# Query scalings of chunk 8 shared between two prologue chunks, and three weight splits in two parts each, in a recurrent attention and two-MoE kernel

## What is computed

```python
# q, k, v, alpha: (4, 8, 768, 48)
for t in range(S):
    state = alpha[:, :, t, :, None] * state + np.einsum('bhd,bhe->bhde', k[:, :, t], v[:, :, t])
    y[:, :, t] = np.einsum('bhd,bhde->bhe', q[:, :, t], state)
# x: (3072, 384) from y
p = domain_probs / (domain_probs.sum(-1, keepdims=True) + 1e-09)
for e in range(4):
    out += p[:, e:e + 1] * (np.maximum(x @ w1[e], 0.0) @ w2[e])
# second block, on out
h = x @ w_in
out = ((h * np.clip(h + 3.0, 0.0, 6.0) / 6.0) @ w_out)
```

## Time and profile before

| what | value |
|---|---|
| time, median of 3 runs | 1395.45 us (1394.85 to 1399.09) |
| time of the profiled execution | 1396.57 us |
| its span | 1394.7 us |
| PE busy | 1371.8 us, 98% of the span |
| POOL busy | 790.4 us, 57% |
| DVE busy | 698.2 us, 50% |
| ACT busy | 534.9 us, 38% |
| mean granted TensorE clock | 0.995 of full |

### The profile page before, as it was taken

How to read it: one execution, slowest core, us unless ns; L and a number is a source line. 1 busy time by engine, 2 the same in 40 slices (tenths; PEclk the granted TensorE clock), 3 DMA queues, 4 the chain that set the end, 5 groups by cost and what they waited for, 6 DMA issues and landing times.

```text
span 1394.7 us, 31927 instructions
## 1 busy us (share of the span) xinstructions
PE 1371.8 (98%) x12476; PEld 1116.7 (80%) x12476; DVE 698.2 (50%) x1401; ACT 534.9 (38%) x992; POOL 790.4 (57%) x860
## 2 busy tenths in 40 slices
PE   7799999999999999999999999999999999999998
PEld 5578888888888888888888888888888888888887
DVE  8766665445454545454544445454445333333333
ACT  2233333333354333354433335533335433335543
POOL 7866666555655565556555655565555444444442
PEclk9899999999999999999999999999999999999999
DMA  4244333343333433333443333343323343333340
GB/s 144 81 133 117 114 117 107 111 116 103 98 98 121 135 106 113 109 94 114 129 120 105 106 98 117 99 138 104 111 84 94 88 132 100 108 98 95 93 123 34
DMA packets 70659, 150.20 MB, mean 108 GB/s; under 512 B 9584, under 2 KB 22128, under 8 KB 70512
## 3 DMA queue, kind: packets, MB, share of 16 engines
q1 hardware_dynamic: 70512, 148.16, 35.6%
HBM read 143.36 MB, written 4.77 MB: 106 GB/s over the span
## 4 chain that ended last, share of the span: by engine, by line
PE 94%; DVE 0%; issue 0%; ACT 0%; DVEq 0%
PE h_bank L469 42%; PE out_banks L485 29%; PE out_third L485 14%; PE score_banks L395 4%; PE score_banks L433 1%; PE score_banks L441 1%; PE state_bank L416 1%; PE state_bank L406 1%; PE h_bank L449 0%; DVE p_kept L577 0%; DVE result L636 0%; DVE h_bank L616 0%; DVE x_lo L632 0%; ACT gate L748 0%; DVEq L141 0%
## 5 line engine op out<-in xcount | busy, mean ns | idle before, releaser
L858 POOL TENSOR_TENSOR w_lo<-w_raw,w_hi 128x768 fp32r<-128x768 f32 x288 | 531.0, 1844 | 551.5 <-ACT w_hi L761 551.5
L755 ACT ACTIVATE h_hi<-h_bank 128x512 fp32r<-128x512 f32 x288 | 172.5, 599 | 636.2 <-DVE h_bank L610 561.4
L469 PE MATMUL h_bank<-x_hi,w_hi 128*128 128x512 f32 x864 | 336.4, 389 | 0.0
L469 PE MATMUL h_bank<-x_lo,w_hi 128*128 128x512 f32 x864 | 336.1, 389 | 0.0
L469 PE MATMUL h_bank<-x_hi,w_lo 128*128 128x512 f32 x864 | 336.0, 389 | 0.0
L610 DVE SCALAR_TENSOR_TENSOR h_bank<-h_bank,probs 128x512 f32<-128x512 f32 x192 | 134.3, 699 | 356.9 <-PE h_bank L469 356.8
L761 ACT ACTIVATE w_hi<-w_raw 128x768 fp32r<-128x768 f32 x288 | 241.4, 838 | 0.0
L485 PE MATMUL out_banks<-h_hi,w_hi 128*128 128x512 f32 x576 | 232.2, 403 | 0.2 <-DVE x_lo L632 0.2
L485 PE MATMUL out_banks<-h_hi,w_lo 128*128 128x512 f32 x576 | 225.0, 391 | 0.0
L485 PE MATMUL out_banks<-h_lo,w_hi 128*128 128x512 f32 x576 | 224.8, 390 | 0.0
L622 DVE TENSOR_TENSOR h_lo<-h_bank,h_hi 128x512 fp32r<-128x512 f32 x288 | 197.3, 685 | 46.5 <-ACT h_hi L755 46.5
(11 more groups left out here) (76 smaller groups left out, 1210.8 us busy)
## 6 DMA issues: line engine op xcount, KB each, us to landing
w_raw<-w SPq DMA_DIRECT2D x288, 384.0 KB, 3.1
alpha_q<-qa SPq DMA_DIRECT2D x48, 256.0 KB, 3.4
k_raw<-kk SPq DMA_DIRECT2D x48, 128.0 KB, 3.4
probs<-prob_scratch SPq DMA_DIRECT2D x24, 256.0 KB, 3.6
v_diag<-v SPq DMA_DIRECT2D x96, 48.0 KB, 2.4
out<-result SPq DMA_DIRECT2D x18, 256.0 KB, 3.9
level_sb<-level SPq DMA_DIRECT2D x1, 80.0 KB, 3.3
ident_sb<-ident SPq DMA_DIRECT2D x1, 64.0 KB, 3.0
```

Of the source, the lines that this page charges most:

```text
L469: mm = pe.matmul(h_bank[g % 2][:, :], a, x, start=k == 0 and i == 0, stop=k == K3 - 1 and i == 2)
L755: act.activation(h_hi[:, g % DEEP, :], h_bank[g % 2][:, :], ACT.Copy).then_inc(hh_made, 1)
L858: pool.tensor_tensor(w_lo[:, g % RING, :], w_raw[:, g % RAW, :], w_hi[:, g % RING, :].bitcast(F32), ALU.subtract).then_inc(w_lo_made, 1)
```

## The change

The seven scalings of chunk 8 used to stand with chunk 6, as the rule "chunk n+2 with chunk n" has it, and none stood with chunk 7. Now steps 0 to 2 stand with chunk 6, ahead of `turn_y(6)`, and steps 3 to 6 with chunk 7: 3, 4 and 5 ahead of `turn_y(7)` and 6 between `turn_y(7)` and `split_x(7)`. Chunks 0 to 5 are as before. In POOL's program `weights_lo(0)`, `(1)` and `(2)` are each two instructions on 128x384 in place of one on 128x768; the semaphore is raised by the second alone. The other 285 are as before.

```diff
             for n in range(PER_TILE):
+                last = n >= PER_TILE - 2
+                ahead = PER_TILE if last else n + 2
+                first, count = (3 * (n - PER_TILE + 2), 3) if last else (0, 4)
                 keep_all(n)
                 next_state(n)
-                for step in range(4 if n + 2 < Q_BEFORE else 0):
-                    scale_q(n + 2, step)
+                for step in range(first, first + count):
+                    scale_q(ahead, step)
                 turn_y(n)
-                if n + 2 < Q_BEFORE:
-                    scale_q(n + 2, 4)
+                if n != PER_TILE - 2:
+                    scale_q(ahead, first + count)
                 split_x(n)
-                for step in range(5, Q_STEPS if n + 2 < Q_BEFORE else 5):
-                    scale_q(n + 2, step)
+                for step in range(first + count + 1, first + count + 1 if last else Q_STEPS):
+                    scale_q(ahead, step)
...
-            def weights_lo(g):
+            def weights_lo(g, parts=1):
 
                 pool.wait_ge(w_hi_made, g + 1)
-                pool.tensor_tensor(w_lo[:, g % RING, :], w_raw[:, g % RAW, :], w_hi[:, g % RING, :].bitcast(F32),
-                                   ALU.subtract).then_inc(w_lo_made, 1)
+                width = PC // parts
+                for i in range(parts):
+                    cols = slice(i * width, (i + 1) * width)
+                    op = pool.tensor_tensor(w_lo[:, g % RING, cols], w_raw[:, g % RAW, cols],
+                                            w_hi[:, g % RING, cols].bitcast(F32), ALU.subtract)
+                op.then_inc(w_lo_made, 1)
...
                 if n == PER_TILE:
-                    weights_lo(0)
-                    weights_lo(1)
-            weights_lo(2)
+                    weights_lo(0, 2)
+                    weights_lo(1, 2)
+            weights_lo(2, 2)
```

## The result

The changed kernel takes 1394.37 us (median of 21 runs, 1393.12 to 1395.84); the kernel before, run beside it, 1396.8 us (21 runs, 1394.68 to 1399.09). The ratio is 0.9984, 95% interval 0.9978 to 0.9991: a gain of 2.2 us, between 1.3 and 3.1 (the two medians differ by 2.4), which is real but under the 0.3% taken as the bound.

A forecast was written before the change was run, and what follows sets the result against it. PE bounds the kernel; only the start of hidden(0) can move, from 75.28 to 74.12, so 1395.45 - 1.16 = 1394.3 us, 0.08% less, no difference that can be told. Eight-in-ten range 1392.8 to 1396.8.

The forecast's parts named there:

- Only the start of `hidden(0)` matters: After the prologue PE runs 1319 us at its own pace; the change only moves when hidden(0) starts, 75.28 us.
- Part 1: Chunk 6: one scaling step fewer ahead of turn_y(6) starts it 0.53 us earlier.
- Part 2: Chunk 6: halved POOL splits give back 0.35 of the 0.65 us won at step 0, turn_y(6) 0.88 earlier in all.
- the price of 0.32 us: POOL's weight splits: halving slots 0 and 1 costs 0.16 us a pair, 0.32 for both.
- starvation: Rival, chance 0.08: POOL's queued instructions keep the port from DVE, hidden(0) near 75.8, 0.5 us slower, 1396.0.
- Part 3: Chunk 7: masked scores start without scalings ahead, matmuls on zeros bind, attend(7) begins at 70.82, 1.87 us earlier.
- Part 4: Before turn_y(7): steps 3 to 5 beside POOL's L843 take about 0.85 us each; turn_y(7) at 72.75, 1.02 earlier.
- "Just so", step 6: Between turn_y(7) and the last x_lo: step 6 ends near 73.58, just ahead of x_lo at 73.62; hidden(0) at 74.12.
- nothing moves: Rival, chance 0.14: step 6 meets the first half of w_lo(2), 0.97 us more, leaving 0.2 us gain, 1395.2.
- The clock: Rival, chance 0.09: PE idle time before carry(7) and hidden(0) lowers the clock; costs 1.3 us, 1395.6, or 1398.

The follow-up runs named there:

- e1: Changed kernel with the three weight splits whole again, so only the scalings of chunk 8 are parted: 1396.07 us against 1396.21 before, ratio 1.0.
- e6: Kernel of e1 (whole splits, parted scalings) with step 6 of chunk 8 behind the last x_lo instead of ahead: 1394.69 us, ratio 0.9994.
- e3: The kernel before, unchanged, run once more for its profile: 1396.33 us (one run).
- e10: The kernel before, unchanged, timed against itself and profiled a third time: 1395.84 us against 1395.94, ratio 0.9999.
- e11: Kernel of e8 with keep_warm(3) in place of keep_warm(5) ahead of attend(7), six matmuls on zeros for ten: 1393.58 us, ratio 0.9981.
- e8: Changed kernel with steps 5, 6 behind the last x_lo and slot 0's w_lo halves moved into POOL's wait for chunk 7's scores: 1393.88 us, ratio 0.9986.

## Why the prediction was right, and where it was not

The time (1394.3 forecast, 1394.37 measured), the range and "no difference of 0.3%" held. The nearness of the first two numbers is luck: the 1.16 us were taken from a median of three runs, 1395.45, where 21 runs gave 1396.8, and inside the 1.16 two errors of about half a microsecond cancelled (parts 3 and 4 below). What can be judged is the difference: 1.16 forecast, 1.33 by the stretches, 2.4 and 1.2 by the two pairs of medians.

- **Only the start of `hidden(0)` matters.** Right: 1319.3 to 1319.5 us behind it in every profile.
- **Part 1, 0.53 us by the order.** Right: with halves in both, 3.23 became 2.64 to 2.71, 0.52 to 0.59; with whole splits 3.27 to 3.36 became 2.83 (e1) and 3.00 (e6).
- **Part 2, the halves give back 0.35.** Right in kind, mis-sized: 0.04 to 0.13 in the old order (3.27 to 3.36 against 3.23), 0.12 to 0.36 in the new one (2.83 and 3.00 against 2.64 to 2.71). The step that failed is the one that let steps 0 and 1 both pass at one boundary as in the earlier trace rows; measured, step 1 took 1.09 and step 2 1.04 us, one step for each half. POOL's splits also started 1.5 us ahead of the mark and not 1.84, so that step 0 slipped in ahead of slot 1's splits. Four halves took 3.97 to 3.99 us and two whole splits 3.59 to 3.72, so the price of 0.32 us for halving slots 0 and 1 was well sized. The rule of the Trainium skill (SBUF — State Buffer, "Who interferes with whom") that the pair is locked for a whole instruction agrees with 1.91 us behind a whole split (e1, e3, e10) and 1.09 behind a half; starvation did not occur.
- **Part 3, `attend(7)` 1.87 us earlier.** 1.25 to 1.68 by the table; against the profile that it was read from, 1.25. Half of the missing 0.62 us is the transpose, 0.56 earlier in place of 0.88, half is the matmuls on zeros. That these would bind is right (e11), but the distance from their first to `attend(7)` is 2.35 us, not the 2.05 that I made of 0.205 a piece; the pace among themselves does not hold for the change to the next kind of matmul.
- **Part 4, the last transpose waits for DVE.** Right in kind, 0.4 us in place of 0.85: the three steps took 2.01 us, 0.67 each. From `attend(7)` to `hidden(0)` it was 2.77 us, where the prediction has 3.30: these 0.53 made up for what part 3 had too much of, and so the sum stood by luck.
- **"Just so", step 6.** This line carried the whole result. The rival "nothing moves" had the mechanism: step 6 behind slot 2's `w_lo`. In the changed kernel the step is ahead by 0.55 us; without the halves it is behind by 0.21, and the whole gain is gone (e1). I had put down the halves to part 2 alone. Their larger effect is that they shift POOL and DVE against each other by 0.8 us at slot 2's split, an accident of timing that e6 replaces by an order that needs none.
- **The clock.** It did not fall in the stretch: from the mark to `hidden(0)` the granted clock was 1.00 in every profile. Ahead of it low stretches lie elsewhere in each execution, and the mark lies between 62.7 and 64.7 us, in both kernels alike.

## What to carry to other kernels

An instruction with two SBUF inputs on DVE should not stand between the last result and the one who waits for it while POOL may be in a long instruction: put it behind, even if the gap looks free. Splitting the long instruction shortens each standstill but makes more of them; moving it into a time in which POOL waits anyway took away more (1.1 us in e8 against 0.1 to 0.4 for the halves), though in e11's execution half of it was lost again. And where a kernel has one moment at which all changes meet, compare profiles from a mark just ahead of the change, not from zero.

## What was not expected of the hardware

The granted clock's low stretches in the prologue fell at different places in executions of the same program, and with them an unchanged point lay up to 2 us apart, more than the whole effect. And PE's standstill of 3.4 us in the midst of chunk 7's scores, for which the profile shows no cause, stands in both kernels, with 3.1 to 4.2 us; no run tried to find its cause.
